# A fused two-layer float32 kernel: TensorE given work from the identity on, a convolution by diagonal matrices, and the second tile turned one step earlier

## What is computed

```
w = exp(weight - max(weight)); w = w / (sum(w) + 1e-9)          # 8 heads x 7 taps
x[b,s,:] = sum_k w[head,k] * x_pad[b,s+k,:]                     # batch 2, seq 4096, 192 features
h = x @ w_in1;  g = h / (1 + exp(-1.702 h));  x = g @ w_out1
h = x @ w_in2;  g = (a0 + a1 h + a2 h^2 + a3 h^3) / (1 + |b0||h| + |b1| h^2 + 1e-6)
out = g @ w_out2
```

## Time and profile before

| | us |
|---|---|
| median of three runs | 1317.78 |
| lowest and highest | 1317.74, 1318.6 |
| the profiled execution, its own time | 1320.08 |
| its span | 1318.3 |
| TensorE busy in the span | 1279.1 (97%) |
| VectorE, ScalarE, GpSimd busy | 1126.2, 1093.1, 533.4 |

### The profile page before, as it was taken

One profiled execution on the slowest core, in us unless ns is written; L12 is line 12 of the kernel. 1 busy time (PEld: TensorE's weight loads), 2 busy tenths in 40 slices (PEclk: granted clock), 3 DMA queues, 4 the chain that ended last, 5 costly groups with the idle time before them and its releaser, 6 DMA issues. The chain is left out here.

```text
span 1318.3 us, 15217 instructions
## 1 busy us (share of the span) xinstructions
PE 1279.1 (97%) x5072; PEld 747.0 (57%) x5072; DVE 1126.2 (85%) x1233; ACT 1093.1 (83%) x1250; POOL 533.4 (40%) x383
## 2 busy tenths in 40 slices
PE   6999999999999999999999999999999999999786
PEld 3556556565665656556565665655556565565432
DVE  6668998989888898988989898898989889777886
ACT  6568898888888888888888888888888888888674
POOL 2414444344443444444444443444434444444221
PEclk9999999999999999999999999999999999999898
DMA  7234445545455554544545454454544555454000
GB/s 183 85 76 114 114 113 132 124 120 136 110 125 117 129 126 115 136 110 124 124 122 134 107 140 113 124 124 109 139 113 124 123 125 116 108 131 105 13 0 24
DMA packets 107822, 148.60 MB, mean 113 GB/s; under 512 B 20961, under 2 KB 45281, under 8 KB 107745
## 3 DMA queue, kind: packets, MB, share of 16 engines
q0 software_dynamic: 33984, 61.88, 27.5%
q1 hardware_dynamic: 73284, 85.75, 19.4%
q10 hardware_dynamic: 477, 0.01, 0.0%
HBM read 13.64 MB, written 6.29 MB: 15 GB/s over the span
## 5 line engine op out<-in xcount | busy, mean ns | idle before, releaser
L961 POOL TENSOR_TENSOR work<-work 128x1024 f32<-128x1024 f32 x127 | 305.1, 2402 | 538.2 <-ACT work L611 491.2
L967 POOL DMA_DIRECT2D g_low<-g_nhi x236 | 207.8, 1015 | 189.8 <-DMA g_low<-g 183.5
L382 PE MATMUL acc_b<-g,down 128*64 128x512 f32 x512 | 248.7, 608 | 11.5 <-DVE g L836 11.4
L362 PE MATMUL acc_a<-g,down 128*128 128x512 f32 x512 | 255.1, 621 | 0.0
L808 DVE TENSOR_TENSOR work<-work,h 128x1024 f32<-128x1024 f32 x128 | 156.3, 1221 | 112.3 <-ACT work L611 110.8
L382 PE MATMUL acc_b<-g,down_b 128*64 128x512 f32 x480 | 231.7, 605 | 0.0
L598 ACT ACTIVATE work<-h,par 128x1024 f32<-128x1024 f32 x128 | 142.5, 1113 | 97.7 <-PE h L356 93.2
L329 PE MATMUL h<-x_a_hi,up_a_hi 128*128 128x512 f32 x510 | 206.8, 406 | 11.1 <-DVE x_a_lo L839 5.5
L331 PE MATMUL h<-x_a_hi,up_a_lo 128*128 128x512 f32 x510 | 199.9, 392 | 0.0
L330 PE MATMUL h<-x_a_lo,up_a_hi 128*128 128x512 f32 x510 | 199.9, 392 | 0.0
L332 PE MATMUL h<-x_b,up_b_hi 128*128 128x512 f32 x510 | 199.6, 391 | 0.0
(11 more groups left out here) (131 smaller groups left out, 1946.7 us busy)
## 6 DMA issues: line engine op xcount, KB each, us to landing
g_low<-g SPq DMA_DIRECT2D x236, 256.0 KB, 2.4
g_low<-g_nhi POOLq DMA_DIRECT2D x236, 256.0 KB, 3.8
out<-y_out SPq DMA_DIRECT2D x15, 384.0 KB, 3.0
x_in<-in_x SPq DMA_DIRECT2D x16, 256.0 KB, 3.1
x_in<-in_x SPq DMA_DIRECT2D x32, 64.0 KB, 2.7
work<-in_moe_w_in SPq DMA_DIRECT2D x8, 256.0 KB, 4.4
work<-in_moe_w_in SPq DMA_DIRECT2D x16, 128.0 KB, 4.6
x_b<-x_hb SPq DMA_DIRECT2D x30, 64.0 KB, 2.1
```

Of the source, the lines that this page charges most:

```text
L362: done = mm(L2.acc_a[:], L2.down[:, f, 0:P], L2.g[:, slot, k, :], start=f == 0, stop=f == STEPS - 1)
L382: return mm(acc_b[l.acc_row:l.acc_row + DB, :], l.down_b[:, f, :], l.g[:, slot, k, :], start=f == 0, stop=f == STEPS - 1)
L961: tt(m, sq[v % 2], seed, ALU.mult).then_inc(m_ready, 1)
L967: pool.dma_start(g_low[:, n % 2, k, :], g_nhi[:, n % 2, k, :], accum_op=ALU.add)\
```

## The change

- TensorE, as soon as the identity is there, multiplies it by itself 12 times (128 columns), ahead of the transposes of tile 0.
- ScalarE makes seven diagonal matrices of 128 by 128, one for each tap of b, by scaling the identity's rows. They lie in a free part of `work`. TensorE convolves b of tile 0 with them: seven matmuls of 256 columns summed in a bank of `L2.h`. VectorE's seven taps of b fall away for tile 0 only. Parts of b are then read from that bank.
- The five products of L533 become three, behind the counts 12, 14 and 16 of `conv_steps`.
- ScalarE rounds b ahead of a, and the second chunk of up weights after both.
- Tile 1 is turned in steps 1 and 2 and no longer in steps 2 and 3. Its convolution stands with 9, 4 and 8 operations in steps 2, 3 and 4, where 3, 7 and 11 stood.
- The two rounds that take the square root of a coefficient (L923 to L926) stand behind steps 0 and 1 on VectorE and no longer ahead of step 0.

```diff
-S_XT_FIRST = (2, 3)
+S_XT_FIRST = (1, 2)
-WARM_AFTER = 9
+WARM_AFTER = (12, 14, 16)
-    CONV_AT_FIRST = (0, 0, 0, 3, 10, NX, NX, NX, NX)
+    CONV_AT_FIRST = (0, 0, 0, 9, 13, NX, NX, NX, NX)
...
+        diagonal = flat[:, 6 * NT * 2:6 * NT * 2 + taps * P].rearrange("p (k d) -> p k d", d=P)
+        first_b = L2.h[:, 0, 0:HALF]
...
             pe.wait_ge(ident_ready, 1)
+            for _ in range(12):
+                mm(L1.acc_a[:, 0:P], ident[:], ident[:], start=True, stop=True)
             transpose_x(0, 0)
             transpose_x(0, 1)
             pe.wait_ge(x_evacuated, 2)
-            pe.wait_ge(conv_steps, WARM_AFTER)
-            for _ in range(5):
+            pe.wait_ge(conv_steps, 1)
+            for k in range(taps):
+                pe.wait_ge(diagonal_ready, k + 1)
+                done = mm(L2.h[:, 0, 0:HALF], diagonal[:, k, :], xt_b[:, k:k + HALF], start=k == 0, stop=k == taps - 1)
+            done.then_inc(first_b_done, 1)
+            for count in WARM_AFTER:
+                pe.wait_ge(conv_steps, count)
                 mm(L1.acc_a[:], ident[:], xt_a[:, HALO:], start=True, stop=True)
...
             evacuate_x(0, 0)
+            act.wait_ge(setup_dve, 6)
+            for k in range(taps):
+                fn(diagonal[:, k, :], ident[:], ACT.Copy, scale=wts[:, 1, k:k + 1]).then_inc(diagonal_ready, 1)
             weights_hi(L1, 0, stage1, w1_hi)
             act.wait_ge(abs_ready, 1)
             fn(root[:, 1:2], root[:, 0:1], ACT.Sqrt).then_inc(setup_act, 1)
             act.wait_ge(setup_act, 3)
             fn(stat[:, 0:1], root[:, 1:2], ACT.Gelu_apprx_sigmoid)
+            x1_b_hi(0)
+            x1_a_hi(0, 0)
             weights_hi(L1, 1, stage1, w1_hi)
-            x1_a_hi(0, 0)
-            x1_b_hi(0)
...
+                def first():
+                    front().then_inc(conv_steps, 1)
+                    keep(halo_a[:, at], xt_a[:, NT:NT + HALO]).then_inc(conv_steps, 1)
+                    keep(halo_b[:, at], xt_b[DB:P, HALF:HALF + HALO]).then_inc(conv_steps, 1)
+                    tap(0, 0).then_inc(conv_steps, 2)
+                    clear(halo_a).then_inc(conv_steps, 1)
+                    clear(halo_b).then_inc(conv_steps, 1)
+                    for k in range(1, taps):
+                        dve.wait_ge(conv_steps, 2 * k + 5)
+                        tap(k, 0).then_inc(conv_steps, 2)
...
-            conv = conv_ops(0)
-            for op in conv[:CONVOLVED]:
-                op().then_inc(conv_steps, 1)
+            first, first_end = conv_ops(0)
+            first()
             dve.wait_ge(w1_hi, 1)
             chunk0_a_lo(0)
             x1_a_lo(0, 0)
+            x1_b_lo(0)
             chunk0_b_lo(0)
-            x1_b_lo(0)
...
+                    if i == 0 and s < 2:
+                        root_round()
```

More of the change, by code:

```diff
@@ L174, in build_program @@
         x_loaded = sem("x_loaded"); x_transposed = sem("x_transposed"); x_evacuated = sem("x_evacuated")
-        conv_steps = sem("conv_steps")
+        conv_steps = sem("conv_steps"); diagonal_ready = sem("diagonal_ready"); first_b_done = sem("first_b_done")
         x1_a_hi_done = sem("x1_a_hi_done"); x1_b_hi_done = sem("x1_b_hi_done")
@@ L565, in x1_b_hi @@
             def x1_b_hi(tile):
-                act.wait_ge(conv_steps, NX * tile + CONVOLVED)
                 if tile == 0:
-                    fn(L1.x_b[0:DB, 0, 0:HALF], conv_b[0:DB, :], ACT.Copy).then_inc(x1_b_hi_done, 1)
-                    fn(L1.x_b[DB:P, 0, HALF:NT], conv_b[DB:P, :], ACT.Copy).then_inc(x1_b_hi_done, 1)
-                    fn(L1.x_b[0:DB, 0, HALF:NT], conv_b[DB:P, :], ACT.Copy).then_inc(x1_b_hi_done, 1)
+                    act.wait_ge(first_b_done, 1)
+                    fn(L1.x_b[0:DB, 0, 0:HALF], first_b[0:DB, :], ACT.Copy).then_inc(x1_b_hi_done, 1)
+                    fn(L1.x_b[DB:P, 0, HALF:NT], first_b[DB:P, :], ACT.Copy).then_inc(x1_b_hi_done, 1)
+                    fn(L1.x_b[0:DB, 0, HALF:NT], first_b[DB:P, :], ACT.Copy).then_inc(x1_b_hi_done, 1)
                 else:
+                    act.wait_ge(conv_steps, NX * tile + CONVOLVED)
                     wait(act, x1_b_moved, 64 * (tile - 1))
@@ L732, in tap @@
                             wait(dve, x1_a_lo_done, tile)
[L733 to L736, removed]
+                        elif tile > 1:
                             wait(dve, x1_hb_done, tile - 1)
@@ L743, in keep, with first_end @@
                     return ts(dst, src, 1.0, None, ALU.mult)
+                def first():
[8 more added lines that the diff above has]
+                        tap(k, 0).then_inc(conv_steps, 2)
+                def first_end():
+                    dve.wait_ge(first_b_done, 1)
+                    dve.wait_ge(conv_steps, CONVOLVED)
+                    keep(xt_a[:, 0:HALO], halo_a[:, at]).then_inc(conv_steps, 1)
+                    keep(xt_b[0:DB, 0:HALO], halo_b[:, at]).then_inc(conv_steps, 1)
                 def clear(halo):
@@ L756, in conv_ops @@
                 assert len(ops) == NX
+                if tile == 0:
+                    return first, first_end
                 def ordered(op, done):
@@ L765, in x1_b_lo @@
                     dve.wait_ge(x1_b_hi_done, 1)
-                    tt(L1.x_b[DB:P, 0, 0:HALF], conv_b[0:DB, :], L1.x_b[0:DB, 0, 0:HALF].bitcast(F32), ALU.subtract)\
+                    tt(L1.x_b[DB:P, 0, 0:HALF], first_b[0:DB, :], L1.x_b[0:DB, 0, 0:HALF].bitcast(F32), ALU.subtract)\
                         .then_inc(x1_b_lo_done, 1)
                     dve.wait_ge(x1_b_hi_done, 2)
-                    tt(L1.x_b[DB:P, 0, HALF:NT], conv_b[DB:P, :], L1.x_b[DB:P, 0, HALF:NT].bitcast(F32), ALU.subtract)\
+                    tt(L1.x_b[DB:P, 0, HALF:NT], first_b[DB:P, :], L1.x_b[DB:P, 0, HALF:NT].bitcast(F32), ALU.subtract)\
                         .then_inc(x1_b_lo_done, 1)
@@ L912, in _, with root_round @@
             x1_a_lo(0, 0)
+            x1_b_lo(0)
             chunk0_b_lo(0)
-            x1_b_lo(0)
-            for op in conv[CONVOLVED:]:
-                op().then_inc(conv_steps, 1)
             chunk0_a_lo(1)
             chunk0_b_lo(1)
-            dve.wait_ge(setup_act, 3)
-            for _ in range(2):
+            first_end()
+            def root_round():
+                dve.wait_ge(setup_act, 3)
                 chain(ts(root[:, 2:3], root[:, 1:2], 1e-18, None, ALU.max))
@@ L926, in _ @@
                 chain(ts(root[:, 1:2], root[:, 2:3], 0.5, None, ALU.mult))
-            ts(root[:, 2:3], root[:, 1:2], 1.0, None, ALU.mult).then_inc(root_ready, 1)
             for i in range(TILES + 2):
@@ L932, in _ @@
                     step(i, s, i % 2, conv, at)
+                    if i == 0 and s < 2:
+                        root_round()
+                    if i == 0 and s == 1:
+                        ts(root[:, 2:3], root[:, 1:2], 1.0, None, ALU.mult).then_inc(root_ready, 1)
         @block.gpsimd
```

## The result

The changed kernel takes 1323.16 us in the median (1320.74 to 1324.95, 9 runs), beside 1317.84 (1317.51 to 1320.10, 9 runs) for the kernel before. It is slower: the ratio is 1.0032, with a 95% interval of 1.0023 to 1.0040, which is 3.0 to 5.3 us: a small loss, but clear of noise. (The ratio is taken from all runs and is not the quotient of the two medians, which is 1.0040.) The profiled execution has a span of 1321.4 us (before 1318.3). The forecast was 1317.7 with a range up to 1320.8.

A forecast was written before the change was run, and what follows sets the result against it. TensorE bounds the kernel, busy nine tenths or more of most slices. Terms: -3.15 at step 6, +0.2 wait left, +2.9 at step 1, sum -0.05, so 1317.7 us, range 1314.8 to 1320.8.

The forecast's parts named there:

- The landing at step 1: Step 1: tile 1's transposes wait for its rows, which land at 24.05; step 2's up-projection 1.38 us late without the clock.
- the start would be hidden behind it: Start: `up_first` ends at 21 to 22.4, ahead of the landing at 24.05, so win or loss there counts nothing.
- The length of the wait: Step 1: TensorE idles 1.7 to 3.1 us, from 21 or 22.4 to 24.1, ahead of tile 1's transposes.
- The clock term: Step 1: the clock falls in the wait for tile 1 and costs 1.5 us, at most 2.7.
- a sign of being wrong: First 80 us: the prediction would be wrong if the clock fell anywhere but between 21 and 29 us.
- The clock's part of the win: Step 6: the low clock behind the `g_low` wait goes too, 1.5 us of the 3.15 to be won.
- Step 5's `g_low` could begin 1.9 us sooner and need no wait: Step 6: convolution operations moved into VectorE's idle time in step 2 remove TensorE's 1.65 us wait, with 0.2 left.
- GpSimd's share: VectorE's idle time ahead of step 3's `g_low`: two GpSimd operations delay VectorE by 1.0 each, 0.56 already paid.
- +1.0 for the sum: Step 6: if VectorE and GpSimd exclude each other, the upper wait of 1.2 holds and the sum is 1.0 higher.
- the wait at step 6 stays: Rival: GpSimd's delays keep step 5's `g_low` late, 3.15 stays and 2.9 is paid: 1320.7 us, chance 0.11.

The follow-up runs named there:

- early_rows: The changed kernel with tile 1's loads put ahead of the third chunk of weights in SyncE's list: 1316.44 us beside 1318.49 for the kernel before, ratio 0.9987.
- turns_only: The kernel before with only tile 1 turned in steps 1 and 2: 1321.02 us beside 1318.49 for the kernel before, ratio 1.0019.
- filled_wait: The changed kernel with five more identity products in the wait for tile 1's rows: 1321.19 us beside 1318.78 for the kernel before, ratio 1.0017.
- spread_only: The kernel before with only tile 1's convolution as 9, 4 and 8 operations in steps 2 to 4: 1319.74 us beside 1318.49, ratio 1.0007.
- before_late_weights: The kernel before with the second layer's up weights converted in steps 4 to 7, not 2 to 5: 1317.26 us beside 1318.78, ratio 0.9986.
- late_weights: The changed kernel with the second layer's up weights converted in steps 4 to 7, not 2 to 5: 1320.89 us, ratio 1.0013 to the kernel before.
- start_only: The changed kernel with tile 1's turns and convolution put back as before: 1317.06 us beside 1318.49 for the kernel before, ratio 0.9989.

## Why the prediction was wrong, point by point

- **The landing at step 1 was right.** The transposes of tile 1 were put at 24.1 with the transfer as releaser; they began at 24.35, released by it. early_rows shows that the landing is the cause, turns_only that it needs no other part of the change. That the start would be hidden behind it holds: alone it is worth 1.4 us, in the changed kernel nothing.
- **The length of the wait was mis-sized.** It was put at 1.7 to 3.1, because the start was thought to bring step 0's end to 21 to 22.4. It was 4.72, from 19.63. The 24 records of the 12 products took 5.11 us, 0.21 each, so the weight load didn't set the pace, and the transposes ended 1.1 us later than before and not 2.4. ScalarE's weights began at 10.73, not 12.0, and its parts of tile 0 ended at 16.49, not 17.9.
- **The clock term was mis-sized.** It was taken at 1.5, upper bound 2.7. The low clock lasted 6.8 us here, 5.6 of them in work, and filled_wait gives its price as 2.5 (from the transposes to step 1's down-projection 5.58, for 3.05 there). With 24.35 for 24.12 that is the whole 1.2 us by which step 2 began later (32.58) than forecast (31.4). The clock also fell in the start, at 9.5, which the forecast named as a sign of being wrong; there it cost little, as TensorE would have waited for ScalarE.
- **The clock's part of the win was probably not there to be won.** The forecast read the 1.5 us of low clock at step 6 from one execution of the kernel before, which took 1320.08 and had a mean granted clock of 0.993. Of the 77 executions of that kernel beside the experiments, 47 have 0.995, as has spread_only's, in which no clock fell in the first 90 us. One low stretch of 3.4 us takes 0.0013 off the mean (an estimate: half of 3.4, by the span). So most executions of the kernel before probably had no fall at step 6, and the median had 1.65 us to give and not 3.15; before_late_weights gave 1.5. This is argued from the mean clocks; no profile of such an execution was kept. It fits the medians, too: they lie 5.3 us apart, where the two profiles lie 4.4 apart at step 8. The nine executions of the changed kernel have 0.989 to 0.992, and its three fastest are the three with 0.992.
- **The step that failed is the one at step 6:** "Step 5's `g_low` could begin 1.9 us sooner and need no wait". It followed one `g_low` and asked whether that one comes in time. The change put three more operations between that of step 2 and that of step 4, the one before it, which had little to spare. In the kernel before, the rows of VectorE and of TensorE for step 4's `g_low` are these:

```profile
45.48 1.22 DVE L849 TENSOR_TENSOR g_low<-g,g_nhi 128x1024 fp32r<-128x1024 f32 x1
```
```profile
47.52 0.50 PE L375 MATMUL acc_a<-g_nhi,down_nhi 128*128 128x512 f32 x1
```

It ended at 46.70 for a use at 47.52: 0.8 us to spare. From the start of step 2's `g_low` to that of step 4 VectorE took 12.1 us before, with 2.15 idle, and 14.9 after, with none. That is 2.8 us more, 0.8 of them spare, and the 2.07 that TensorE waited.

- **GpSimd's share was counted for one step.** The forecast had one pair of its operations in the way. There are three pairs between the two `g_low`, and each delays two VectorE operations: six delays, 6.1 us together, where the kernel before has 2.6 (the first taps, 1.50 and 1.38 for 0.49 and 0.35, and 0.55 of the `g_low` at 38.60). So of the 4.95 us that VectorE works longer (14.9 for 9.95), 3.5 are GpSimd's and the three added operations are the other 1.4. late_weights shows that without GpSimd's six the same 16 operations leave no wait. The rule of "SBUF — State Buffer" ("Who interferes with whom") in the Trainium skill, that the two engines exclude each other for a whole instruction, was the better guide: it was weighed with +1.0 for the sum and needed to be applied to each pair.
- **The rival "the wait at step 6 stays"** (0.11) came nearest, and its 1320.7 was low: it had the wait as it was and the clock term at 1.5. Measured at step 8: +1.2 from step 1 beyond the forecast, +1.9 of wait (2.07 for 0.2), +1.5 of clock (3.3 us at half clock behind it), together 4.6 over a forecast of nothing, for the 4.4 seen.
- **The parts and the whole.** By the medians start_only, turns_only and spread_only come to -1.4, +2.5 and +1.3, in sum +2.4, where the whole is +3.0 to +5.3. With about 1.3 us of interval on each part, the sum may still be the whole. The start's 1.4 us should be missing from the whole, as it is lost behind the landing. That it also makes the wait longer (4.72 for 3.22 in turns_only), and the low clock behind it 6.8 us instead of 3.4, is seen in one profile of each and is not shown for the median.

## What to carry to other kernels

Work that is moved ahead of a wait is worth what the next landing leaves of it: read the landing of each transfer that the moved instruction needs, and move the transfer in its queue before moving the instruction. When operations are spread over steps to clear one late result, check every result that the new places stand ahead of, with its own spare time; the neighbour with the least decides. And where VectorE and GpSimd work side by side, count each GpSimd operation as a delay in each step, and try first to move GpSimd's work out of the crowded steps: one line did here what the rearranged convolution didn't. Before a low clock of one profiled execution is counted as time to be won, see in the mean clock of the other executions whether it is usual.

## What the runs showed of the hardware

- The clock behind a wait differs between executions. It fell behind waits of 1.63 and 1.65 us (start_only, before) and of 2.07 (the changed kernel), and it was granted in full behind a wait of 2.07 in spread_only and in early_rows. At the start it fell behind a wait of 1.93 in the changed kernel and not behind one of 1.98 in early_rows. A low clock lasted 3.4 us in before and turns_only, 6.8 in the changed kernel and 10.2 in late_weights, in which TensorE was busy without a gap from 24.03 on. The term of 1.5 us for a fall was one draw of several.
- Each of the six late VectorE operations began inside one of GpSimd's and ended 0.02 to 0.56 us behind its end, small or large: the copy of 64x6 at 39.90 ended at 41.03, GpSimd's of 39.70 at 41.00. So the six delays are about 1 us each (0.96 to 1.08), for GpSimd's operations of 1.3 and more. It goes the other way, too: GpSimd's operation at 44.78, issued while `g_low` of 44.33 ran, took 1.89 for 1.28. The Trainium skill ("SBUF — State Buffer", "Who interferes with whom") has it that of two that want the shared pair of ports the later one to issue is fully blocked; these rows agree.
- The 24 float32 records of the identity's products (128 columns each) took 5.11 us in the changed kernel, 0.21 each. That is the pace of 1.2 GHz: a record of 512 columns took 0.85 in the start before. So a fresh weight load for each record cost nothing over the time of its columns. The granted clock reads 1.00 in this stretch (1.5 to 6.6), so in the first microseconds the pace has to be read from the rows.
